# Eight small tiles move from the top of the on-chip memory to a place below the large scratch tiles

## The reference, cut to what matters

```python
# 1: attention of tokens over states, and of states over tokens, for every batch and head
a = softmax(x @ state.T / 8);   xread = a @ state
a2 = softmax(state @ x.T / 8);  sread = a2 @ x
x = rows of [xread; sread]                      # 2176 x 512
# 2: dense block, hidden width 2048
h = x @ w_in;  x = (h - tanh(h)) @ w_out
# 3: eight experts of hidden width 1024, all rows through all of them
P = exp(x @ w_gate - max), then 8 times: rows, then columns scaled to their sums
out = sum over e of P[:, e:e+1] * (relu(x @ w1[e]) @ w2[e])
```

## Time and profile before

| | us |
|---|---|
| median of 3 runs | 1875.1 |
| lowest and highest run | 1874.64 and 1877.22 |
| the profiled execution | 1877.22 |
| its span, first to last instruction | 1875.4 |
| mean granted TensorE clock | 0.997 |

### The profile page before, as it was taken

One profiled execution on the slowest core, in us unless ns is written; L12 is line 12 of the kernel. 1 busy time (PEld: TensorE's weight loads), 2 busy tenths in 40 slices (PEclk: granted clock), 3 DMA queues, 4 the chain that ended last, 5 costly groups with the idle time before them and its releaser, 6 DMA issues.

```text
span 1875.4 us, 20899 instructions
## 1 busy us (share of the span) xinstructions
PE 1855.6 (99%) x8409; PEld 1533.4 (82%) x8409; DVE 615.5 (33%) x1013; ACT 413.1 (22%) x750; POOL 59.9 (3%) x58
## 2 busy tenths in 40 slices
PE   7999999999999999999999999999999999999999
PEld 5888888888888888888888888888888888888887
DVE  6656665621452113211321232123211321142121
ACT  6434344421121112111211121112111211121111
POOL 4200000310000000000000000000000000000000
PEclk9899999999999999999999999999999999999999
DMA  6101101110020002000200020002000200010001
GB/s 230 45 1 45 45 0 51 46 40 1 0 63 29 0 1 63 29 1 0 69 22 1 0 73 18 1 0 74 18 1 0 74 18 1 0 46 23 1 28 45
DMA packets 28231, 56.41 MB, mean 30 GB/s; under 512 B 5104, under 2 KB 5104, under 8 KB 27248
## 3 DMA queue, kind: packets, MB, share of 16 engines
q1 hardware_dynamic: 28144, 55.08, 9.2%
HBM read 50.61 MB, written 4.46 MB: 29 GB/s over the span
## 4 chain that ended last, share of the span: by engine, by line
PE 97%; DVE 1%; issue 1%; ACT 1%; POOL 0%; DVEq 0%; ACTq 0%; POOLq 0%
PE bank L1128 12%; PE bank L1130 12%; PE bank L1129 12%; PE bank L1142 12%; PE bank L1143 12%; PE bank L1144 12%; PE bank L1097 3%; PE bank L1098 3%; PE bank L1099 3%; PE bank L1081 1%; PE bank L1083 1%; PE bank L1082 1%; PE bank L1037 1%; PE bank L1070 1%; PE bank L1173 1%
## 5 line engine op out<-in xcount | busy, mean ns | idle before, releaser
L763 DVE SCALAR_TENSOR_TENSOR hl<-bank,hh 128x512 fp32r<-128x512 f32 x256 | 177.1, 692 | 952.8 <-ACT hh L538 952.8
L1128 PE MATMUL bank<-xh,w1h 128*128 128x512 f32 x1024 | 400.4, 391 | 0.2
L538 ACT ACTIVATE hh<-bank 128x512 fp32r<-128x512 f32 x256 | 153.1, 598 | 1116.2 <-PE bank L1130 1116.2
L1130 PE MATMUL bank<-xh,w1l 128*128 128x512 f32 x1024 | 398.7, 389 | 0.0
L1142 PE MATMUL bank<-w2h,hh 128*128 128x512 f32 x1024 | 398.5, 389 | 0.0
L1129 PE MATMUL bank<-xl,w1h 128*128 128x512 f32 x1024 | 398.5, 389 | 0.0
L1144 PE MATMUL bank<-w2h,hl 128*128 128x512 f32 x1024 | 398.4, 389 | 0.0
L1143 PE MATMUL bank<-w2l,hh 128*128 128x512 f32 x1024 | 398.3, 389 | 0.0
L1128 PEld LDWEIGHTS bank<-xh,w1h 128*128 128x128 f32 x1024 | 192.3, 188 | 40.8 <-issue 1.3
L1130 PEld LDWEIGHTS bank<-xh,w1l 128*128 128x128 f32 x1024 | 192.2, 188 | 40.3
L1142 PEld LDWEIGHTS bank<-w2h,hh 128*128 128x128 f32 x1024 | 192.2, 188 | 40.0
(11 more groups left out here) (129 smaller groups left out, 1372.0 us busy)
## 6 DMA issues: line engine op xcount, KB each, us to landing
st<-w SPq DMA_DIRECT2D x160, 256.0 KB, 2.7
xT<-xT SPq DMA_DIRECT2D x8, 512.0 KB, 8.0
xn<-xn SPq DMA_DIRECT2D x4, 1024.0 KB, 6.0
out<-yacc SPq DMA_DIRECT2D x3, 1024.0 KB, 3.9
out<-yacc SPq DMA_DIRECT2D x5, 256.0 KB, 2.1
sT<-sT SPq DMA_DIRECT2D x2, 128.0 KB, 3.3
wg_raw<-wg SPq DMA_DIRECT2D x1, 16.0 KB, 2.4
```

Of the source, the lines that this page charges most:

```text
L538: nc.scalar.activation(hh[:, f % NH], hpsum[f % NH][:], ACT.Relu).then_inc(s_hh, 1)
L763: v.scalar_tensor_tensor(hl[:, f % NH], hpsum[f % NH][:], 0.0, hh[:, f % NH].bitcast(f32), ALU.max, ALU.subtract).then_inc(s_hs, 1)
L1128: mm(out, w1h[:, f, k, :], xh[:, k, own_rows(c)], start=(k == 0), stop=False)
L1130: last = mm(out, w1l[:, f, k, :], xh[:, k, own_rows(c)], start=False, stop=(k == KT - 1))
```

## The change

The eight small tiles are laid out before `hiddens` and no longer after `end`. `wg_raw` (128 bytes) now stands ahead of `wg`. No instruction, wait, loop or shape differs; only the addresses of operands do.

```diff
@@ build, the layout @@
         place[0] = after_acc
 
+        ident = sb("ident", [P, P])
+        pr = sb("pr", [P, E, TQ])
+        gcur = sb("gate_now", [P, TQ])
+        rsum = sb("rsum", [P, TQ])
+        csum = sb("csum", [P, E])
+        call = sb("call", [P, E])
+        gmax = sb("gmax", [P, 1])
+        amax = sb("amax", [P, 1])
+
         hiddens = place[0]
         hh = sb("hh", [P, NH, S], f32r)
@@
         place[0] = scratch
+        wg_raw = sb("wg_raw", [P, KT, E])
         wg = sb("wg", [P, KT, P], f32r)
-        wg_raw = sb("wg_raw", [P, KT, E])
         lg_rows = sb("lg_rows", [2 * E, T])
@@
         assert place[0] <= scratch
-
-        place[0] = end
-        ident = sb("ident", [P, P])
-        pr = sb("pr", [P, E, TQ])
-        gcur = sb("gate_now", [P, TQ])
-        rsum = sb("rsum", [P, TQ])
-        csum = sb("csum", [P, E])
-        call = sb("call", [P, E])
-        gmax = sb("gmax", [P, 1])
-        amax = sb("amax", [P, 1])
-        assert place[0] <= nc.sbuf_usable_end, (place[0], nc.sbuf_usable_end)
+        assert end <= nc.sbuf_usable_end, (end, nc.sbuf_usable_end)
```

## The result

The changed kernel takes 1911.3 us (1910.88 to 1911.7, 4 runs) against 1876.16 us (1874.64 to 1878.2, 4 runs): a ratio of 1.0185, with a 95% interval of 1.0173 to 1.0198. It is slower by 35 us. The forecast was no change, and the measured time lies outside the stated range of 1870 to 1881 us.

What follows compares the result with a forecast made beforehand. The prediction took TensorE, busy 99% of the span at 226.7 ns a matmul, as the bound. Every term was nothing: 1877.2 us for the profiled execution plus nothing, stated as the median 1875.1 us, range 1870 to 1881.

Steps and rivals of the forecast that it cites:

- I take nothing: TensorE's streamed operands: 768 dense-block matmuls and 8 of the logits stream a moved tile without cover; cost put at zero.
- I cost them at nothing; what hides a slower load is that slack: TensorE's held operands: 3,592 matmuls hold a moved one; loads of 188 ns leave 38.7 ns free; cost zero.
- The signs of being wrong: L1142 above 228 ns beside 226.7 at L1128, L1097 above 231, no clock dip, or ScalarE/VectorE lengths changed over 5%.
- matmuls with and without a moved operand now run at one pace: TensorE before the change: 226.7 ns for both kinds in the experts, so no gain was expected from moving operands.
- my argument against the rival: state_up streams w1h in four 512-byte pieces at the same 389 ns as unbroken streams, so beginning anew costs nothing visible.
- VectorE's scalar in the earlier trace: L901: VectorE reads a gate at 4-byte steps, in every phase, in 750 to 752 ns; nearest row for taking zero.
- the side for which there was no evidence but absence: Whole kernel: no change, within 0.2% or 3.75 us, including the rival of engines meeting in memory; chance 0.86.
- A shifted stream costs TensorE time: Rival, slower: moved operands in L1097 to L1099 and L1142 to L1144 cost time; 1880.6 or 1906.1 us; chance 0.09.
- held as well: The shifted-stream rival's case where held operands pay besides streamed ones: 1875.1 + 31.0 = 1906.1 us; chance 0.04.
- The transfer of `sT`: Load at the start: lands at 6.0 us, TensorE's first matmul at 9.56, so 3.5 us hide it; cost nothing.
- what the prediction feared of such pieces: sT load: 128-byte pieces for the first half of the partitions would cross 256-byte multiples, slowing it by less than double.
- the clock's dip: TensorE's clock at half from about 50 to 61 us; rival: its loss gives 1870.9 us (0.04), a second dip 0.01.

Runs made afterwards that it cites:

- e3: The kernel before the change with start raised by 32 bytes, so that every tile stands 32 bytes off a multiple of 64: 1874.77 us.
- f3: The kernel before the change with only w2h and w2l (and the tanh and state-token tiles inside them) moved by 32 bytes: 1910.47 us.
- f4: The kernel before the change with xh and xl laid out ahead of w2h, and w2h, w2l and all behind them 32 bytes further: 1893.54 us.
- e2: The kernel before the change, small tiles still at the top, with 32 bytes left free below hiddens: 1907.15 us.
- e4: The kernel before the change with 64 bytes left free below hiddens: 1907.75 us.
- e1: The changed kernel with hiddens and all behind it padded by 32 bytes to multiples of 64 (moved by 1,408 bytes): 1908.18 us, ratio 1.0165.
- f1: The kernel before the change with 128 bytes left free below hiddens: 1908.79 us.
- h1: The kernel before the change with only hh and hl shifted, by 16 bytes, as slices of larger tiles: 1881.84 us.
- h2: The kernel before the change with only hh and hl shifted, by 4 bytes, as slices of larger tiles: 1906.5 us.
- h3: The kernel before the change with hiddens and all behind it 192 bytes further: 1890.48 us.
- g3: The changed kernel with 160 bytes of padding behind the small tiles, so that hiddens moves by 1,536 bytes: 1876.92 us, ratio 1.0001.

## Why the prediction was wrong

**The step that failed** is "I take nothing", for the streamed operand, and "I cost them at nothing; what hides a slower load is that slack", for the held one. The runs put in their place a price for a stream and a load that stand in different phases modulo 256 bytes: 5.7 to 7.5 ns a matmul on average at eleven of the sixteen entries of the table that are off 0, and 0, 2.2, 3.0, 4.5 and 9.5 ns at the rest. In the change it is 7.5 ns in down and 6.8 in dense down, 27.5 us together, and 2.8 us for the states. The signs of being wrong that the prediction had named came true: L1141 at 234.2 ns, and dense down at 234.2.

**Why the slack hid nothing.** The load did take 188 ns as before, with 38.7 ns to spare, and the pace fell nevertheless. The price is not a longer load: e3, f3 and f4 show that it hangs on the places of the streamed and the held tiles against each other. Within one kind of matmul this could be a stream and the load for the next matmul, which run at once, or a stream and its own operand, which was loaded before it. The steps from up to down in e2 decide: the matmul before the step streams `xh` and holds `w1l`, both unmoved, only the load beside it is of a moved tile, and the step takes 235 ns. It is so at 4 and 128 bytes as well (235, and 231 to 233), while at 64 and 96 the price comes only in the steps behind it. That the two accesses get in each other's way in the memory is my reading of this; the runs show on what the time depends, not the conflict itself. Slack of a busy time was no cover here.

**Why the rows did not show it.** That "matmuls with and without a moved operand now run at one pace" was right, and said nothing: in the kernel before all these pairs have d = 0. For the same reason my argument against the rival was empty: the four pieces of 512 bytes that state_up streams keep the phase modulo 256. The same goes for VectorE's scalar in the earlier trace rows: it is another engine's, and one value per partition, not a stream beside a load. I had named this gap ("no row shows a stream that starts 32 bytes off a multiple of 64") and still gave 0.86 to the side for which there was no evidence but absence.

**The rival that came near.** "A shifted stream costs TensorE time", held as well, gave 1906.1 us at a chance of 0.04. Its size is near by accident: 7.1 ns from one more unit of 64 bytes, where 7.5 and 6.8 are measured. Its mechanism is wrong: e3 shifts every stream and costs nothing, e4 and e1 keep multiples of 64 and cost nine tenths of it. It also missed the 3.6 us of up and dense up, whose operands stay: after a stretch out of phase TensorE needs some matmuls to settle. In the changed kernel, in the 139 whole groups of twelve up matmuls behind a down group, the first takes 232.8 ns on average, the second 231.0, and from the third on it is within 0.4 ns of 226.7, but for the last with 227.8. At other distances this costs more: up lost 5.7 us in e1, 5.8 in f1 and 6.0 in f3, a sixth to a fifth of each loss, though none of its pairs is shifted.

**Two rules beside the runs.** The Trainium skill ("SBUF — State Buffer", Specifications) gives lines of 16 bytes, and by these a move of 86 lines is free: here it cost 35 us. h1 against h2 (down free at 16 bytes, 5.7 ns at 4) is compatible with lines of 16 playing a part, but at 32, 64, 96 and 128 bytes, all multiples of 16, down pays 5.7 to 7.5 ns. The Trainium skill ("TensorE: Matmul & The Clock Gate", Part 2: What happens when you issue a matmul) has the stream and the load on two independent read ports and says that loading the next weights doesn't steal from the running matmul. The traces disagree: with the same loads of 188 ns beside it, a stream comes every 226.7 or every 234.2 ns, by the places of these two against each other.

**What was right, and what was only likely.** The transfer of `sT` was hidden, as were its 0.6 us. Its pieces of 128 bytes for one half of the partitions now cross multiples of 256. In the six runs in which one half's pieces do (the change, e2, e3, e4, f4 and h3) the median from issue to landing is 3.6 to 3.9 us, in the other ten 3.3 to 3.6. So what the prediction feared of such pieces is borne out in its direction, but the two ranges touch, and the other half's transfer, whose pieces cross nothing, is as late; no run parts the two. The other engines' lengths, the small tiles' own place and the clock's dip did not matter. The count of matmuls with a moved operand left out attention's (`sT`, `a2T` and others); by their starts they changed by less than 0.2 us.

**What stays open.** Why this period, why +16 and 192 cost little or nothing, and why the price begins at once at 32 bytes and a step later at 64 and 96, is not settled: no run shows how the memory is divided, or when within a matmul the two accesses fall. Whether a distance between the measured ones is better than 0 wasn't tried, nor was a shift of less than 32 bytes on any tile but `hh` and `hl`.

## What to carry to other kernels

Where TensorE is the bound and changes its held operand with every matmul, lay out all tiles that it holds or streams at one phase modulo 256 bytes, and pad small tiles to 256 ahead of them: 160 bytes were worth 1.8% here (g3). When a change moves only addresses, look at which pairs of accesses run at once, and don't read equal paces as proof that places don't matter while all places in the trace share one phase. Slack in one access did not hide what it did to the other: a cover must be checked for what the two parties share. And a stretch that keeps its own places can still lose, because it begins in the state that the stretch before it left.

## What the runs showed of the hardware

In these runs a float32r stream of 512 columns with a load of 128 beside it comes every 226.7 ns at 2.4 GHz if both stand in one phase modulo 256 bytes. At most other distances tried it comes every 232 to 237 ns on average. The exceptions are 16 bytes ahead, which is free, 192, which costs 2 to 3 ns, and 240, which costs 4.5. Back in one phase the pace settles at 226.7 after one matmul (e2), after two (the change), or after five to seven (f4, e1, f1, f3).

In this kernel and its variants the median from issue to landing of `sT`, two transfers in pieces of 128 bytes, was 3.6 to 3.9 us where one half's pieces crossed multiples of 256 bytes, and 3.3 to 3.6 us where none did.
